# Queries of a fused attention and routed-MLP kernel: loaded in rows of 32 values and turned by VectorE

## What is computed

```python
kv = np.einsum('bhsd,bhse->bhde', k, v)
out = np.einsum('bhsd,bhde->bhse', q, kv)
rms = np.sqrt(np.mean(out * out, axis=-1, keepdims=True) + 1e-06)
x = out / rms * g_norm            # to 4608 tokens x 512
h = np.maximum(x @ w_in, 0.0)     # 512 -> 2048
x = (h * h) @ w_out               # 2048 -> 512
# expert e = argmax(x @ w_gate + modality_bias[modality_id]), 8 experts
out = gate * (np.maximum(x @ w1[e], 0.0) @ w2[e])   # 512 -> 1024 -> 512
```

## Time and profile before

| | |
|---|---|
| median of three runs | 1389.92 us |
| the profiled execution | 1391.38 us |
| its span | 1389.6 us |
| VectorE busy | 785.5 us, 57% |
| ScalarE busy | 593.5 us, 43% |
| GpSimd busy | 499.9 us, 36% |
| mean granted TensorE clock | 0.994 |
| DMA packets | 183397, 237.44 MB |

### The profile page before, as it was taken

How to read it: one execution, slowest core, us unless ns; L and a number is a source line. 1 busy time by engine, 2 the same in 40 slices (tenths; PEclk the granted TensorE clock), 3 DMA queues, 4 the chain that set the end, 5 groups by cost and what they waited for, 6 DMA issues and landing times. The chain is left out here.

```text
span 1389.6 us, 20776 instructions
## 1 busy us (share of the span) xinstructions
PE 1364.2 (98%) x6951; PEld 1113.1 (80%) x6951; DVE 785.5 (57%) x1693; ACT 593.5 (43%) x1201; POOL 499.9 (36%) x589
## 2 busy tenths in 40 slices
PE   5999999999999999999999999999999999999997
PEld 5888888888888888888887887877787888888876
DVE  3456574574563663664664655556655555565555
ACT  3443334334243333333343333334555555555553
POOL 2643232222132222232232234504555555555551
PEclk9999999999999999999999999999999999999999
DMA  8644646657566556567464465779995113851270
GB/s 225 184 111 149 197 119 195 191 120 207 182 130 206 172 145 200 164 131 223 151 152 157 145 146 169 192 256 207 345 377 173 47 45 131 298 192 49 70 261 20
DMA packets 183397, 237.44 MB, mean 171 GB/s; under 512 B 58734, under 2 KB 101646, under 8 KB 183314
## 3 DMA queue, kind: packets, MB, share of 16 engines
q1 hardware_dynamic: 169010, 214.85, 52.3%
q0 software_dynamic: 9472, 19.96, 4.5%
q10 hardware_dynamic: 4832, 1.57, 0.5%
HBM read 148.07 MB, written 89.30 MB: 171 GB/s over the span
## 5 line engine op out<-in xcount | busy, mean ns | idle before, releaser
L669 POOL TENSOR_TENSOR stage<-stage,stage_hi 128x512 f32<-128x512 f32 x128 | 170.7, 1334 | 548.9 <-ACT stage_hi L1149 548.7
L1494 DVE TENSOR_TENSOR g_sb<-g_sb 128x512 f32<-128x512 f32 x144 | 101.9, 708 | 324.0 <-ACT g_hi L1213 316.5
L1211 ACT ACTIVATE g_sb<-ps_h 128x512 f32<-128x512 f32 x144 | 86.1, 598 | 427.8 <-PE ps_h L816 227.5
L814 PE MATMUL ps_y<-g_hi,weights 128*128 128x512 f32 x576 | 231.0, 401 | 0.0
L814 PE MATMUL ps_h<-xT_hi,weights 128*128 128x512 f32 (+1 forms) x580 | 230.6, 398 | 0.0
L816 PE MATMUL ps_h<-xT_hi,weights 128*128 128x512 f32 (+1 forms) x580 | 226.0, 390 | 0.0
L815 PE MATMUL ps_h<-xT_lo,weights 128*128 128x512 f32 (+1 forms) x580 | 225.5, 389 | 0.0
L816 PE MATMUL ps_y<-g_hi,weights 128*128 128x512 f32 x576 | 224.9, 390 | 0.0
L815 PE MATMUL ps_y<-g_lo,weights 128*128 128x512 f32 x576 | 224.6, 390 | 0.0
L1239 ACT ACTIVATE kv_sb<-ps_h 32x256 f32<-32x256 f32 x456 | 171.1, 375 | 119.8 <-PE ps_h L1001 114.4
L742 POOL DMA_INDIRECT k_sb<-rows,v_sb x148 | 148.5, 1003 | 83.5 <-issue 46.4
(11 more groups left out here) (269 smaller groups left out, 1735.5 us busy)
## 6 DMA issues: line engine op xcount, KB each, us to landing
stage<-in_moe_w SPq DMA_DIRECT2D x128, 256.0 KB
w_hi<-stage_hi SPq DMA_DIRECT2D x128, 256.0 KB
w_lo<-stage SPq DMA_DIRECT2D x128, 256.0 KB
weights<-w_hi SPq DMA_DIRECT2D x32, 1024.0 KB
weights<-w_lo SPq DMA_DIRECT2D x32, 1024.0 KB, 6.5
rows<-y_sb SPq DMA_DIRECT2D x36, 256.0 KB
q_sb<-in_q SPq DMA_DIRECT2D x28, 256.0 KB, 3.2
k_sb<-in_k SPq DMA_DIRECT2D x28, 160.0 KB, 3.5
```

What stands on the lines that cost most here:

```text
L669: pool.tensor_tensor(stage[n % 2][:, :], stage[n % 2][:, :], stage_hi[n % 2][:, :].bitcast(F32), ALU.subtract).then_inc(split_lo, 1)
L814: pe.matmul(out_ap, lhs[0], rhs[0], start=start, stop=False)
L1211: act.activation(g_sb[:, :], ps_h[c % 2][:, 0:GROUP], ACT.Relu).then_inc(h_read, 1)
L1494: dve.tensor_tensor(g_sb[:, :], g_sb[:, :], g_sb[:, :], ALU.mult).then_inc(g_done, 1)
```

## The change

The queries from the second group on are no longer loaded as whole rows of 64 values. `fetch_q_blocks` loads, for each pair of heads and each quarter of 32 values in it, the tokens of a part in blocks of 32: partition p of a quarter holds token p of each block, and a block is 32 columns. One instruction of VectorE that transposes blocks of 32 by 32 then gives `tile_T` as it was. TensorE's transposes, their PSUM bank and ScalarE's copy go. A part is 16 DMAs of 32 partitions, with runs of 128 bytes, in two halves in two chunks of SP's order. The third tile of a group goes to a part of `v_sb` instead of `q_sb`, with its own semaphore. The first "qT" of a group moves from place 12 to 8. Waits are moved as needed: `heads` takes those that `qT` had for PSUM and kv, `load_q` waits for VectorE's transposes, `load_kv` for the third tile's.

```diff
@@ ATTEND
-              (12, "qT", 0), (14, "heads", 0), (17, "xT", 0),
+              (8, "qT", 0), (14, "heads", 0), (17, "xT", 0),
@@
+        q_blocks = [q_sb[:, :], q_sb[:, :], v_flat[1][:, 0:D], q_sb[:, :]]
@@
-        ps_qT, ps_heads, ps_xT = (ps_a, ps_a, ps_b, ps_a), (ps_b, ps_a, ps_b, ps_a), (ps_b, ps_a, ps_b, ps_a)
+        ps_heads = ps_xT = (ps_b, ps_a, ps_b, ps_a)
@@
+        def fetch_q_blocks(eng, a, t, hp, signal):
+            for batch, lo, hi in q_parts(a, t):
+                first_row = a.c * GROUP + t * P + lo - batch * S
+                for i in range(4):
+                    head, d = PAIR * hp + i // 2, i % 2 * QUAD
+                    rows = q[batch:batch + 1, head:head + 1, first_row:first_row + hi - lo, d:d + QUAD]
+                    eng.dma_start(q_blocks[t][i * QUAD:(i + 1) * QUAD, hp * P + lo:hp * P + hi].rearrange("p (j d) -> p j d", d=QUAD),
+                                  rows.rearrange("b h (j p) d -> p (b h j) d", p=QUAD)).then_inc(signal, 16)
@@ sync
             def load_kv(a, hp):
                 sp.wait_ge(kv_ps, a.count(HP, hp - 1))
+                if hp == 1 and a.c > 1:
+                    sp.wait_ge(qT_done, a.count(TILES, -1))
...
-            def load_q(a, t):
-                sp.wait_ge(qT_ps, a.count(TILES, t))
-                fetch_q(sp, a, t, q_sb, q_in)
+            def load_q(a, t, hps):
+                sp.wait_ge(heads_ps, TILES)
+                sp.wait_ge(qT_done, a.count(TILES, (0, 1, 0, 2)[t]))
+                if t == 2 and a.c < B:
+                    sp.wait_ge(kv_ps, a.count(HP, HP))
+                for hp in hps:
+                    fetch_q_blocks(sp, a, t, hp, q_in[t == 2])
@@
-                        if c == Q_AT[t]:
-                            load_q(a, t)
+                        if c in Q_AT[t]:
+                            part = Q_AT[t].index(c) * HP // 2
+                            load_q(a, t, range(part, part + HP // 2))
@@
-            KV_AT, Q_AT, ROWS_AT = (0, 0, 3, 3), (2, 6, 8, 10), 11
+            KV_AT, Q_AT, ROWS_AT = (0, 0, 3, 3), ((1, 2), (5, 6), (7, 8), (9, 10)), 11
@@ tensor
-            def qT(a, t):
-                pe.wait_ge(q_in, q_loaded(a, t))
-                if t == 0:
-                    if a.c < B:
-                        pe.wait_ge(kv_done, a.count(1, 1))
-                elif t == 1:
-                    pe.wait_ge(qT_done, a.count(TILES, 1))
-                else:
-                    pe.wait_ge(x_lo_done, a.count(TILES, t - 1))
-                for k_ in range(KC):
-                    last = pe.transpose(chunks(ps_qT[t][:, :])[:, k_, :], q_sb[:, k_ * P:(k_ + 1) * P], ident[:, :])
-                last.then_inc(qT_ps, 1)
-
             def heads(a, t, route):
                 pe.wait_ge(qT_done, a.count(TILES, t + 1))
-                if t == 0 and route:
-                    pe.wait_ge(prefix_read, a.shifted(-2).count(1, 1))
-                    pe.wait_ge(gate_spread, a.shifted(-2).count(1, 1))
+                if t == 0:
+                    pe.wait_ge(kv_done, min(a.c + 1, B))
+                    if route:
+                        pe.wait_ge(prefix_read, a.shifted(-2).count(1, 1))
+                        pe.wait_ge(gate_spread, a.shifted(-2).count(1, 1))
+                elif t >= 2:
+                    pe.wait_ge(x_lo_done, a.count(TILES, t - 1))
@@ scalar
-                if what == "qT":
-                    act.wait_ge(qT_ps, a.count(TILES, n + 1))
-                    if n:
-                        act.wait_ge(heads_ps, a.count(TILES, n))
-                    elif route:
-                        act.wait_ge(logits_ps, r.count(1, 1))
-                    act.activation(tile_T[:, :, :], chunks(ps_qT[n][:, :]), ACT.Copy).then_inc(qT_done, 1)
-                elif what == "heads":
+                if what == "heads":
@@ vector
+                elif what == "qT":
+                    dve.wait_ge(q_in[n == 2], q_loaded(a, n))
+                    dve.wait_ge(heads_ps, a.count(TILES, n))
+                    if n == 0 and route:
+                        dve.wait_ge(logits_ps, r.count(1, 1))
+                    dve.transpose(tile_T[:, :, :].rearrange("p k t -> p (k t)"), q_blocks[n]).then_inc(qT_done, 1)
```

More of the change, by code:

```diff
@@ L305, in routed_mlp_program @@
         const_in, mod_in = sem("const_in"), sem("mod_in")
-        q_in, kv_in = sem("q_in"), [sem(f"kv_in{n}") for n in range(2)]
+        q_in, kv_in = [sem(f"q_in{n}") for n in range(2)], [sem(f"kv_in{n}") for n in range(2)]
         stage_in = [sem(f"stage_in{n}") for n in range(2)]
@@ L407, in q_loaded @@
         def q_loaded(a, t):
-            return 16 * sum(len(q_parts(Group(c), n)) for c in range(1, a.c + 1) for n in range(TILES if c < a.c else t + 1))
+            per_part = 16 * 4 * HP
+            return per_part * sum(len(q_parts(Group(c), n)) for c in range(1, a.c + 1) for n in range(TILES if c < a.c else t + 1)
+                                  if (n == 2) == (t == 2))
         FIRST_KV = HP * 32 - HP // 2 * 16
@@ L931, in other @@
                     kv(a, n)
-                elif what == "qT":
-                    qT(a, n)
                 elif what == "heads":
```

## The result

The changed kernel takes 1415.37 us (median of 4 runs, 1412.76 to 1419.35) against 1390.64 us before, measured on the same chip (4 runs, 1389.65 to 1391.58): a ratio of 1.0176, with a 95% interval of 1.0164 to 1.0188. So it is slower by 25 us. The prediction had the sign right and the size wrong: it said 1396, and the measured time lies above its whole range of 1379 to 1411. The profiled execution has a span of 1417.6 us, 28.0 more than before.

A forecast was written before the change was run, and what follows sets the result against it. The prediction took TensorE, busy 98% of the span, as the bound. Its sum was -14.7 + 4.8 + 7.7 + 8.2 = +6.0 us, 1397.4 against 1391.38, or 1396 as a median; the range was 1379 to 1411.

The forecast's parts named there:

- the spanning tiles' batches in groups 2, 4 and 6: Tiles over two batch rows take 32 DMAs on SP, delaying weight pieces and relus: +2.3, +1.2, +4.7, together +8.2 us.
- TensorE saves 14.7 us: On TensorE, 32 blocks of four query transposes go, at 0.46 us a block: -14.7 us.
- VectorE's turns: 32 transposes of 128x512 on VectorE, partly on the g chain, stall 0 to 1.3 us a group; 0.6 taken, +4.8 us.
- An ordinary tile's batches cost nothing: On SP, 8 DMAs ahead of the load in each of two chunks are hidden: price 0, up to 0.7 us a DMA.
- The pitch, 0.57: Time SP takes per small query DMA: 0.57 us, between 0.46 (list loads) and 0.65 (64-partition loads).
- if 0.46, everything moves to rival 1: Sign in SP's timeline afterwards: batches at a pitch of 0.46, not 0.57, would point to the faster outcome.
- rival 1: Faster, 1379 us: pitch 0.46, VectorE's transposes fall into GpSimd's waits, ScalarE's idle time swallows late pieces; chance 0.26.
- The k and v loads of later groups: On SP, up to 4 us later behind the queries of chunks 1 and 2, but they have that much: price 0.
- Group 0, 7.7 us: First tile's 32 DMAs on SP delay k and v; the last v lands at 68.7, TensorE used it near 61.05: +7.7 us.
- some tenths of slack: TensorE's heads matmuls may wait for tile 2's turned queries, with some tenths of slack; counted inside the VectorE bound.
- Rival 3: Much slower, 1431 us: a batch of 8 outlasts its chunk, from 0.7 us a DMA; chance 0.11.
- rival 4: Queries come late, so TensorE waits for them in place of transposing; 1400 to 1410 us, chance 0.05.

The follow-up runs named there:

- e5: Changed kernel with 2 query DMAs a part and VectorE turning only 32 of 512 columns; 1415 us, groups 1 to 7 1.72 to 1.93 us shorter than before.
- e9: Kernel before with only the new query loads, second and fourth tiles' into v_sb; groups 0, 2, 4, 6 +8.64, +6.46, +9.39, +9.31 us.
- e1: Changed kernel with one DMA for each block of 32 tokens, 16 for every tile; 1393.84 us against 1392.87 before, ratio 1.0016.
- e3: Changed kernel with 2 query DMAs for a part of a tile, not 16, the rest not loaded; 1387.57 us, ratio 0.9958.
- e7: Changed kernel with 8 DMAs of the first tile's second part left out in group 0, 24 ahead of v; group 0 1.60 us slower than before.
- e4: Kernel before with queries by 16 DMAs of 64 partitions a part, all in one chunk; 1569.41 us, ratio 1.125.
- e13: Changed kernel with each small DMA moving 16 of its 32 values; groups 0, 2, 4, 6 +7.68, +6.47, +4.01, +6.00 us against before.
- e14: Changed kernel with a DMA per block of 32 tokens, ScalarE issuing 4 of a tile's 16, SP 6 and 6; 1383.96 us against 1389.65 before, ratio 0.9957.

## Why the prediction was right and wrong

The step that failed is the price of the spanning tiles' batches in groups 2, 4 and 6: the prediction had 8.2 us together, the trace has 21. The terms in turn:

- **TensorE saves 14.7 us.** Right: 1.82 us a group measured in groups 1 to 7 with the turns nearly gone (e5), against 1.84.
- **VectorE's turns, 4.8 us, 0.6 a group.** Nearly right: 0.83 a group, 6.6 in all, inside the bounds of 0 to 1.3. A turn takes 0.70 us, as the earlier trace rows said.
- **An ordinary tile's batches cost nothing.** Right at best: 0.00 in groups 1, 3 and 5 of e9. It isn't so in every execution, as the medians of e1 and e3 say, 6.3 us apart. Group 7 shows how: +3.09 in the changed kernel, -0.78 in e7. In the first a load was issued 8.0 us after the first scatter and in the second 4.6 us, and the split of the piece waited 5.01 and 2.54 us for it; in the first TensorE then waited 2.13 us for `xn` and ran on at half the clock. That the batches make a load meet the scatters so is argued from these two traces. The k and v loads of later groups, also priced at 0, were free: TensorE waited for none.
- **The pitch, 0.57.** It was 0.475, the lower of the two bounds, that of the short list loads. DMAs of 32 partitions by four runs of 128 B took 0.43 us, those of 64 partitions by one run of 256 B 0.60 (e4, medians), in the same queue. With it, the prediction's own formula gives less loss, so the pitch is not what made it too low. The sign that it gave for this case, "if 0.46, everything moves to rival 1", misled.
- **Group 0, 7.7 us.** The mechanism was right: SP's queue, v late, TensorE idle. The idle was 5.45 us. What was missing is the price of the idle itself: 3.7 us more in a stretch at half the granted clock. No term of the sum had that. That 7.7 came out near the true 9.1 is luck: the pitch, taken too high, made up 2.2 of the 3.7 us that were missing.
- **Spanning tiles in groups 2, 4 and 6, 8.2 us together.** This is the failed step. Measured against the ordinary -1.0 a group, they cost 8.3, 6.2 and 6.8, which is 21 us. The place and the direction were right, and four things were left out. First, each batch was laid on the timeline of before, as if SP came to it on time. In group 2 its first batch began at 270.47, which is 263.9 on the clock of the group before the change, and not at 260.20: the batches of chunks 1 and 2 and the eight k and v loads of chunk 3 had already made it late, and these I had priced at 0. Second, the lateness was let go after two chunks. A batch of 8 with its pieces takes SP 5.4 us (289.82 to 295.26 for load, stores and batch), in a chunk of 6.8. So lateness is worked off by 1.4 us a chunk at most, and some was still there when the scatters came. There a late store or load becomes a very late one (the store landed after 7.7 us and the load after 7.1 in group 2, the load after 9.2 in group 6). Third, the heads product waits for the turn, which on VectorE stands behind the late relu: 2.46 us in group 2 and 5.26 in group 6, where the prediction had "some tenths of slack". Fourth, these idles too were followed by stretches at half the clock, 1.6 us in group 2. What each of the four is worth was not separated by a run.
- **The rivals.** None of them happened as a whole. Rival 1's pitch came true, and its claim that ScalarE's idle time swallows late pieces holds at best for batches of 8 and not for 16. Rival 3's mechanism was real, a batch that outlasts its chunk, but I had tied it to a pitch of 0.7 and not to the 32 DMAs of a spanning tile, which outlast theirs at 0.475: 7.6 us and more, in chunks of 6.5. It was in my rows. VectorE waited for the queries themselves (rival 4) once, 2.2 us, in group 0.
- **The Trainium skill** ("DMA: Bandwidth & Descriptors", Bandwidth), from whose times for 4 and 64 KB the prediction estimated 0.74 us for one transfer, by which transport would set the pace: the trace disagrees for these, 0.475 us apart, and half the bytes changed nothing (e13). The page's times are for DMAs that GpSimd issued, and these are SP's.

The sum as measured in the profiled execution: -14.7 + 6.6 for all eight groups, + 9.1 for group 0, + 21.3 for groups 2, 4 and 6, + 4.1 for group 7 and + 1.1 for groups 1, 3 and 5, each against the ordinary -1.0 a group: 27.5, where the groups of the two profiled executions differ by 27.4. It must close, since the last terms are what is left of each group; it shows where the 21.5 us stand that the prediction's 6.0 lacks: 13.1 in groups 2, 4 and 6, 5.2 in groups without a spanning tile, 1.8 at VectorE's turns and 1.4 in group 0.

## What to carry to other kernels

Price small DMAs by their place: count how many stand ahead of each transfer that somebody needs, and carry the queue's lateness forward from chunk to chunk until it is worked off, rather than laying each batch on the timeline of before. Look at the worst case of the loop (here the tile in two parts) first, since the ordinary one was nearly free and the worst one cost 30 us. Where idle time of TensorE is in the sum, ask also what clock it will have behind it. To repair the loss, cut the number in the worst case and share the rest with a queue whose engine idles: 12 on SP and 4 on ScalarE gave 0.4% where 32 on SP lost 1.8%.

## What the runs showed of the hardware

- An idle of TensorE can cost more than its length. In group 0 it idled 4.53 and 0.92 us and ran at a granted clock of 0.50 (the 1.2 GHz level) from then until 71.83, and matmuls of 128x512 started 0.43 us apart, not 0.23. After 2.27 us of idle in two pieces (e7) the clock stayed at 1.00. The length doesn't decide alone: in the changed kernel 2.46 us left it at 1.00 and 2.13 us were followed by 0.50.
- About 25 of the 576 small DMAs took 0.6 to 2.1 us to issue and not 0.43, 22 us in all, at fairly regular distances. Of these 16 start within 0.3 us of packets of 16 KB on the queue that the profile's page calls "instruction" (46 in the run). That the one causes the other is argued from the times alone; no run tested it.
- A DMA that ScalarE issues holds it as long as SP: 0.48 us apart in e14 against 0.475.
- Behind the four scatters of the token list, three of SP's transfers of 256 KB took 7.1 to 9.2 us to land (store at 312.29, loads at 320.04 and 723.78); in the two chunks ahead of the scatters of group 2 it was 2.9 to 3.4.
